# Attention kernel: rows of x and their gate products from one product of 96 columns, with the partial sums of the logits added by VectorE

## The reference, cut to what matters

```python
for t in range(S):
    y[:, :, t] = np.einsum('bhd,bhde->bhe', rt, state)
    Sa = np.einsum('bhde,bhe->bhd', state, at)
    state_decay = state * wt[:, :, None, :] - np.einsum('bhd,bhe->bhde', Sa, bt)
    state = state_decay + np.einsum('bhd,bhe->bhde', vt, kt)
...
x = np.ascontiguousarray(attn_out.transpose(0, 2, 1, 3)).reshape(B * S, H * D)
...
logits = x @ w_gate
noise_scale = np.log1p(np.exp(x @ w_noise))
noisy_logits = logits + noise_scale * noise
```

## Time and profile before

| | |
|---|---|
| median of 3 runs | 1591.04 us (1590.13 to 1598.68) |
| the profiled execution, its own time | 1593.16 us |
| its span, first to last instruction | 1591.4 us |
| TensorE busy | 1440.8 us, 91% |
| VectorE, ScalarE busy | 578.8 us, 587.5 us |
| mean granted clock of TensorE | 0.911 of 2.4 GHz |
| attention | from 0 to about 569 us |

### The profile page before, as it was taken

How to read it: one execution, slowest core, us unless ns; L and a number is a source line. 1 busy time by engine, 2 the same in 40 slices (tenths; PEclk the granted TensorE clock), 3 DMA queues, 4 the chain that set the end, 5 groups by cost and what they waited for, 6 DMA issues and landing times.

```text
span 1591.4 us, 45341 instructions
## 1 busy us (share of the span) xinstructions
PE 1440.8 (91%) x19945; PEld 1115.7 (70%) x19945; DVE 578.8 (36%) x1107; ACT 587.5 (37%) x1167; POOL 293.0 (18%) x263
## 2 busy tenths in 40 slices
PE   2889989899898727999999999999699999999999
PEld 2778878788787626888888888888435555555556
DVE  6665565564643260000000000000165445445441
ACT  1555364453544321111211112111176545554451
POOL 5532233232220001111111111111320010000000
PEclk9787797876878657999999999999799999999999
DMA  3223232222311177555555555556410011000000
GB/s 117 61 87 94 68 105 74 80 82 73 92 44 35 52 228 248 185 170 172 168 181 183 170 170 168 185 178 203 128 50 21 26 32 31 25 17 9 13 9 21
DMA packets 87553, 161.20 MB, mean 101 GB/s; under 512 B 39552, under 2 KB 53888, under 8 KB 87360
## 3 DMA queue, kind: packets, MB, share of 16 engines
q1 hardware_dynamic: 79776, 132.41, 26.5%
q0 software_dynamic: 7584, 25.90, 5.3%
HBM read 141.39 MB, written 16.88 MB: 99 GB/s over the span
## 4 chain that ended last, share of the span: by engine, by line
PE 60%; DMA 1%; issue 1%; DVE 0%; ACT 0%; POOL 0%; POOLq 0%; DVEq 0%
PE pY L1027 15%; PE pY L1169 13%; PE pH L1008 13%; PE pH L1156 11%; PE pH L1013 4%; PE pH L1159 3%; PE pX L997 1%; PE pX L1144 1%; PE pX L998 0%; DMA xs<-x,slot_token 0%; DMA rows<-results,pos 0%; POOL rows L1135 0%; DVE down L1244 0%; DMA results<-ys 0%; ACT mxT L1198 0%
## 5 line engine op out<-in xcount | busy, mean ns | idle before, releaser
L1027 PE MATMUL pY<-down,hT 128*128 x880 | 245.9, 433 | 0.0
L1008 PEld LDWEIGHTS pH<-exT,up 128*128 128x128 f32 x1760 | 207.9, 194 | 11.5 <-issue 1.7
L1053 ACT ACTIVATE hT<-pH 128x512 f32<-128x512 f32 x110 | 59.7, 594 | 419.4 <-PE pH L1013 419.4
L1061 DVE COPY ys<-pY 128x320 f32<-128x320 f32 x55 | 27.0, 492 | 507.1 <-PE pY L1027 507.1
L1008 PE MATMUL pH<-exT,up 128*128 128x128 f32 x1760 | 208.5, 277 | 2.5 <-ACT exT L1046 2.5
L1169 PE MATMUL pY<-wout,down 128*128 128x320 f32 x768 | 210.4, 433 | 0.0
L1027 PEld LDWEIGHTS pY<-down,hT 128*128 128x128 f32 x880 | 163.0, 190 | 61.2
L1169 PEld LDWEIGHTS pY<-wout,down 128*128 128x128 f32 x768 | 144.3, 190 | 60.7 <-issue 3.0
L1156 PE MATMUL pH<-mxT,win 128*128 128x512 f32 x384 | 172.5, 603 | 4.9 <-ACT mxT L1198 4.7
L1156 PEld LDWEIGHTS pH<-mxT,win 128*128 128x128 f32 x384 | 73.8, 193 | 91.6 <-issue 82.2
L988 POOL DMA_DIRECT2D results<-ys x55 | 31.9, 580 | 428.4 <-DVE ys L1061 428.4
(11 more groups left out here) (189 smaller groups left out, 2146.0 us busy)
## 6 DMA issues: line engine op xcount, KB each, us to landing
up<-in_moe_w SPq DMA_DIRECT2D x55, 1024.0 KB, 5.2
up_rest<-in_moe_w SPq DMA_DIRECT2D x110, 128.0 KB, 5.1
down<-in_moe_w SPq DMA_DIRECT2D x8, 1280.0 KB, 14.3
results<-ys POOLq DMA_DIRECT2D x55, 160.0 KB
wfr<-in_wdec SPq DMA_DIRECT2D x32, 240.0 KB
kbT<-in_kb SPq DMA_DIRECT2D x32, 240.0 KB
uv<-in_vt SPq DMA_DIRECT2D x16, 312.0 KB, 3.8
aT<-in_at SPq DMA_DIRECT2D x16, 240.0 KB
```

Of the source, the lines that this page charges most:

```text
L1008: pe.matmul(pH[t % 2][b][:, c, :], up[t % NU][:, k, f * P:(f + 1) * P], xT[t % 2][:, k, :], start=(c == 0 and k == 0), stop=False, skip_gr ...
L1027: m = pe.matmul(pY[t % 2][:, 0:D], hT[t % 2][:, j, :], down[:, bass.ds(e, 1), j, :].rearrange("q n d -> q (n d)"), start=(j == 0), stop=(j ...
L1053: nc.scalar.activation(hT[t % 2][:, b * HT:(b + 1) * HT, :], pH[t % 2][b][:], ACT.Relu).then_inc(h_copied[b], 1)
```

## The change

The transposes and the gate products become one. A tile `xw` holds, for each pair, 96 columns: 80 columns of an identity (40 for each head) and the 16 gate columns. TensorE multiplies each 128 tokens of a pair of `yT` by it, six products (12 records) for an X, and both the rows and this pair's part of the logits land in PSUM. The products of the two pairs aren't accumulated in PSUM any more: ScalarE copies the rows, and VectorE then adds the parts of the logits, two instructions of 128x48 for an X, of which the second waits for the first. VectorE waits for ScalarE to have finished its two copies. X is thereby taken by two engines, and whoever waits for its slot waits for both. The store of the rows waits for ScalarE only. At the start VectorE fills the identity part of `xw` with two copies.

```diff
-            by, n = count[tok, g]
-            eng.wait_ge(act_done if by == "act" else dve_done, n)
+            for by, n in count[tok, g]:
+                eng.wait_ge(act_done if by == "act" else dve_done, n)
...
             def store(g, half):
-                taken(sp, f"X{half}", g)
+                sp.wait_ge(act_done, count[f"X{half}", g][0][1])
...
                 elif kind == "X":
                     taken(pe, f"Y{half}", g)
+                    if g == 0:
+                        pe.wait_ge(gate_loaded, 16)
+
                     for i in range(2):
                         for j in range(W // P):
-                            pe.transpose(out[:, i, cols(j, P)], yT[:, i, cols(j, P)], ident[:])
-
-                    if g == 0:
-                        pe.wait_ge(gate_loaded, 16)
-                    else:
-                        taken(pe, tok, g - 1)
-                    first, odd = g // 2 * (S // P) + half * (W // P), g % 2 == 1
-                    if odd:
-                        pe.matmul(out[:, 0, W:W + W // P * 2 * E], ident[:], logits[:, first:first + W // P, :].rearrange("q c n -> q (c n)"),
-                                  start=True, stop=False, skip_group_check=True)
-                    for j in range(W // P):
-                        for i in range(2):
-                            m = pe.matmul(out[:, 0, W + j * 2 * E:W + (j + 1) * 2 * E], yT[:, i, cols(j, P)], gw[:, g % 2 * 2 + i, :],
-                                          start=(i == 0 and not odd), stop=(i == 1), skip_group_check=True)
+                            m = pe.matmul(out[:, i, cols(j, DD + 2 * E)], yT[:, i, cols(j, P)], xw[:, g % 2 * 2 + i, :], start=True, stop=True)
...
                     for i in range(2):
-                        copy(xr[:, i, rows, :].rearrange("q c (h d) -> q c h d", d=D),
-                             t[:, i, 0:W].rearrange("q (c h d) -> q c h d", h=2, d=64)[:, :, :, 0:D])
-                    first = g // 2 * (S // P) + half * (W // P)
-                    m = copy(logits[:, first:first + W // P, :], t[:, 0, W:W + W // P * 2 * E].rearrange("q (c n) -> q c n", n=2 * E))
+                        m = copy(xr[:, i, rows, :], t[:, i, 0:W // P * (DD + 2 * E)].rearrange("q (c n) -> q c n", n=DD + 2 * E)[:, :, 0:DD])
...
+                elif kind == "X":
+
+                    dve.wait_ge(act_done, count[tok, g][0][1])
+                    first = g // 2 * (S // P) + half * (W // P)
+                    to = logits[:, first:first + W // P, :]
+                    of_pair = [t[:, i, 0:W // P * (DD + 2 * E)].rearrange("q (c n) -> q c n", n=DD + 2 * E)[:, :, DD:DD + 2 * E] for i in range(2)]
+                    if g % 2 == 1:
+                        after_step(nc.vector.tensor_tensor(to, of_pair[0], to, ALU.add))
+                        m = nc.vector.tensor_tensor(to, of_pair[1], to, ALU.add)
+                    else:
+                        after_step(nc.vector.tensor_copy(to, of_pair[0]))
+                        m = nc.vector.tensor_tensor(to, of_pair[1], to, ALU.add)
...
+            for h in range(2):
+                nc.vector.tensor_copy(xw[:, :, h * D:(h + 1) * D], ident[:, 64 * h:64 * h + D].unsqueeze(1).to_broadcast([P, 4, D]))
```

More of the change, by code:

```diff
@@ L94, in attention @@
                 continue
-            by = "act" if split(tok)[0] in BY_ACT else "dve"
-            ends[by] += 1
             number[tok, g] = len(number)
-            count[tok, g] = by, ends[by]
+            count[tok, g] = []
+            for by in ("act", "dve") if tok[0] == "X" else ("act",) if split(tok)[0] in BY_ACT else ("dve",):
+                ends[by] += 1
+                count[tok, g].append((by, ends[by]))
     in_order = list(number)
@@ L146, in attention @@
         identh = sb("identh", [P, P], BF16)
-        gw = sb("gw", [P, 4, gate_w.shape[2]])
+        xw = sb("xw", [P, 4, DD + 2 * E])
         slot = [ctx.enter_context(nc.psum_tensor(f"wide{b}", [P, 2, 512], F32)) for b in range(3)]
@@ L260, in _ @@
             load_v(0, 1)
-            sp.dma_start(gw[:], gate_w).then_inc(gate_loaded, 16)
+            sp.dma_start(xw[:, :, DD:DD + 2 * E], gate_w).then_inc(gate_loaded, 16)
             sp.wait_ge(pads_set, 4)
@@ L624, in over_pairs, with after_step @@
                 return mask[:].rearrange("q c f -> q (c f)").unsqueeze(1).to_broadcast([P, 2, W])
+            steps = [0]
+            def after_step(ins):
+                steps[0] += 1
+                ins.then_inc(scan_step, 1)
+                dve.wait_ge(scan_step, steps[0])
             def take(tok, g):
@@ L651, in take @@
                 m.then_inc(dve_done, 1)
[L653 to L659, removed]
             def make_decays(g, i):
@@ L722, in _ @@
                         hop += 1
-                    elif tok[0] != "J" and split(tok)[0] not in BY_ACT:
+                    elif tok[0] == "X" or tok[0] != "J" and split(tok)[0] not in BY_ACT:
                         take(tok, g)
```

## The result

The changed kernel takes 1578.57 us (median of 4 runs, 1572.24 to 1585.77) beside 1591.17 for the kernel before: a ratio of 0.9899, with an interval of 0.9869 to 0.9928. On another occasion it took 1579.37 (7 runs), a ratio of 0.9915 (0.9881 to 0.9949). So it is faster by 0.9 to 1.0%, some 13 to 16 us. The profiled execution took 1582.93 us.

What follows compares the result with a forecast made beforehand. TensorE, with a chain of hops woven in, was taken to bound attention's loop. Durations saving 6.3 us plus the clock's 16 gave 22.3 us less, 1569 us against the median 1591.04; range 1552 to 1586.

Steps and rivals of the forecast that it cites:

- part of the spells gone: Attention loop: some lower-clock stretches after X0 vanish, 12 to 32 us less, 1559 to 1579 us; chance 0.45.
- The stretch before a fall: TensorE around X0: same work before all seven clock falls, including waits of 0.6 for `yT` and 0.69 for `uv`.
- The work of X: TensorE in X: 12 records of 96 columns take 1.38 us, saving 0.64 or 0.89 each, 12.2 us in all.
- The bound from the 128-column products of the experts: Record time in X: the experts' fp32 products take 0.118 us each, so X takes at most 1.42 us.
- The new wait: Behind X1, VectorE's additions delay `u` to T+1.5, T being X's end on TensorE: 3.8 us lost, plus 1.7 in the drain.
- The sum without the clock: Whole kernel: X's saving less the waits and the start copies, 12.2 - 3.8 - 1.7 - 0.4 = 6.3 us less.
- The clock, 16 us less: Attention: denser X avoids some lower-clock stretches after X0; 16 us taken, bounds 0 and 35, at 0.31 per us there.
- What is spent again: TensorE at full clock also waits for instructions, up to 2.2 us at once, and such waits can bring new falls.
- All the spells go: Rival: all seven lower-clock stretches after X0 vanish, 41 us less, 1550 us; chance 0.15.
- The pattern stays: Rival: the waits or later steps cause the falls, so only durations count, 6.3 us less, 1585 us; chance 0.28.
- Falls after X1: Rival: the added wait behind X1 in the loop drops the clock, up to 5 us each, 1615 us; chance 0.07.

Runs made afterwards that it cites:

- sixteen columns: Changed kernel with each product of X streaming only the 16 gate columns, the other 80 left out; 1591.11 us, ratio 1.0004 to the kernel before.
- VectorE's part alone: Kernel before, transposes and narrow products kept, but each pair's product in its own place and added by VectorE; 1596.42 us, ratio 1.0028.

## Why the prediction came out as it did

The time, 1578.6, lay within the range of 1552 to 1586 and 10 us above the 1569 forecast; the case that came, part of the spells gone, was the likeliest. Its steps one by one:

- **The stretch before a fall.** The prediction found it the same in all seven cases, two waits included. It isn't. X0 of group 1 has no wait ahead of it, and F1, the step behind X0 of group 4, already runs in 0.53 us and not in 0.38: the fall at 376.6 comes before the hop and its wait. So the rows of before already spoke against the waits as the cause. X0 of group 1, from the timeline of TensorE before:

```profile
180.95 0.87 PE L491 MATMUL wide<-ident,yT 128*128 128x128 f32 x6
```

- **The work of X.** Mis-sized by a little: the 12 records took 1.51 us where 1.38 was taken, 0.126 for each and not 0.112 to 0.118. X saves 0.51 and 0.76, 10.2 us over 16 and not 12.2. The bound from the 128-column products of the experts was too low, for a reason that no run shows; in the same place sixteen columns took 0.117 and not 0.112 either.
- **The new wait.** Right: `u` at T+1.50, as forecast, additions of 0.21 each, `st` at T+1.21 for T+1.24. VectorE's part alone cost 4.5 us, expected 3.9.
- **The sum without the clock, 6.3 us less.** With X as measured it is 4.3. Adding the durations and treating the clock as a separate term was the weak step: with sixteen columns, where X is as short as the prediction had it, the kernel is 0.6 us slower than before (3.0 less to 4.3 more), since the mean clock fell from 0.80 to 0.77. That kernel's X is also emptier than before, so it shows that the two terms depend on each other, and not that the shorter step is worth nothing.
- **The clock, 16 us less.** Right in its mechanism: sixteen against ninety-six columns is 14 to 17 us, and the long stretches fell from seven to two. As the prediction's own term it was too high: of the 13 to 16 us measured, 9 to 12 are left behind the 4.3 of the durations. Its two factors were off in opposite directions. At 0.31 for each, 16 us are 52 us fewer at the lower level; over the six turns there were 65 fewer, and they gave 0.15 each. That the number came so near is in part luck.
- **What is spent again.** Named, not sized: the waits of which the profile names no releaser rose by 19 us. They account for one turn that is longer than before at the same clock.
- **The rivals.** "All the spells go" was wrong by the two left, and its 41 us overlooked these waits. "The pattern stays" is excluded by the five that went although the waits stayed (0.59 and 0.66 us at X0 of group 2); the sixteen columns, which keep the seven, gave 1591 and not 1585. "Falls after X1" did not happen: behind each of the six X1 of the loop the clock of the changed kernel is 1.00 for 8 us.

So the 13 to 16 us measured are about 4 for the durations and 9 to 12 for the clock, if the two are added as the prediction did. What is shown more firmly is that with 16 columns in place of 96, and all else equal, nothing of them is left.

## What to carry to other kernels

Where a profile shows TensorE falling to its lower clock behind the same step each time, look at how empty the array is in that step, not only at how long it takes: here 96 columns in place of 16 under the same weight loads cost 0.1 us a step and gave 14 to 17 us, while a step as short with 16 columns gave nothing against before. When work moves to another engine, put it behind the take-up of a hop that others wait for: the same two additions made `u` wait until T+1.50 ahead of it and not at all behind it, some 9 us over the kernel with an uncertainty of 5. And expect the next limit to appear as the clock rises, so that a microsecond freed from the lower level is worth less than a single turn suggests: here 0.15 us and not 0.3, while waits that the profile puts down to nothing rose from 25 to 44 us. The supply of instructions is a likely cause of these, not a shown one.

## What the runs showed of the hardware that was not expected

- X with 12 records of 16 columns and no transposes was followed by a long stretch at the lower level seven times of seven (1.0004); with 96 columns under the same weight loads by two and one (0.9899, 0.9915).
- Adding 12 us of useless streaming (ordinary products for transposes) left the time unchanged, 0.9997, while the clock's mean rose from 0.80 to 0.88.
- Waits of TensorE for which the profile names nothing grew with its clock, from 22 to 30 us at a mean of 0.77 to 0.82 to 38 to 46 us at 0.87 to 0.90, and leaving out a third of the loads didn't change them (44.8 us).
- An fp32 record of 96 columns with its 128-column weight load took 0.126 us, of 16 columns 0.117 (1.41 over 12) in the same place.
